# Attention and an MLP on one core: a third product with v in three passes, and what makes room for it

## The reference

```python
q_rot, k_rot = (rotate(q), rotate(k))                 # q, k, v: 4 x 8 heads x 576 x 64, fp32
scores = scale * np.matmul(q_rot, k_rot.transpose(0, 1, 3, 2))
scores = scores - np.max(scores, axis=-1, keepdims=True)
attn = np.exp(scores)
attn = attn / (np.sum(attn, axis=-1, keepdims=True) + 1e-09)
x = np.matmul(attn, v)                                # to (2304 tokens, 512)
h = x @ w_in                                          # 512 x 1024
e = np.exp(h - np.max(h, axis=-1, keepdims=True))
solu = h * e / (np.sum(e, axis=-1, keepdims=True) + 1e-09)
ln = (solu - mu) / np.sqrt(var + 1e-06) * g_ln
out = ln @ w_out                                      # 1024 x 512
```

## Time and profile before

| what | us |
|---|---|
| median of 3 runs | 485.28 (484.88 to 485.31) |
| the profiled execution's own time | 485.69 |
| its span | 483.6 |
| PE busy in the span | 474.4 |
| DVE busy | 375.4 |
| ACT busy | 263.7 |
| POOL busy | 221.7 |

### The profile page before, as it was taken

One profiled execution on the slowest core, in us unless ns is written; L12 is line 12 of the kernel. 1 busy time (PEld: TensorE's weight loads), 2 busy tenths in 40 slices (PEclk: granted clock), 3 DMA queues, 4 the chain that ended last, 5 costly groups with the idle time before them and its releaser, 6 DMA issues.

```text
span 483.6 us, 7879 instructions
## 1 busy us (share of the span) xinstructions
PE 474.4 (98%) x2555; PEld 402.4 (83%) x2555; DVE 375.4 (78%) x592; ACT 263.7 (55%) x398; POOL 221.7 (46%) x283
## 2 busy tenths in 40 slices
PE   7899999999999999999999999999999999999997
PEld 6678888988898888889888878888888888888885
DVE  6867887888879788878886366999997899888731
ACT  4667787777787778877786343032224222322221
POOL 6778565757575756666571012343343121122110
PEclk9999999999999999999999999999999999999999
DMA  8403455545454555445434203233333223322232
GB/s 289 186 18 76 139 159 112 175 136 169 101 152 150 150 143 148 148 115 179 123 80 100 58 15 58 32 82 67 86 69 80 47 50 69 84 54 62 60 78 86
DMA packets 101008, 50.60 MB, mean 105 GB/s; under 512 B 90280, under 2 KB 90280, under 8 KB 99048
## 3 DMA queue, kind: packets, MB, share of 16 engines
q1 hardware_dynamic: 100152, 50.00, 38.6%
q10 hardware_dynamic: 816, 0.10, 0.1%
HBM read 33.33 MB, written 4.79 MB: 79 GB/s over the span
## 4 chain that ended last, share of the span: by engine, by line
PE 94%; DVE 2%; DMA 1%; ACT 1%; issue 0%; SPq 0%; DVEq 0%; ACTq 0%
PE ps L1145 20%; PE ps L1159 20%; PE ps L1131 19%; PE ps L1082 18%; PE ps L1053 8%; PE ps L1111 5%; PE ps L1097 4%; DMA X<-x_in 1%; DVE nm L822 1%; DVE QK L797 1%; ACT p_main L633 0%; DVE X L763 0%; ACT QK L580 0%; DVE w_lo L846 0%; DVE X L768 0%
## 5 line engine op out<-in xcount | busy, mean ns | idle before, releaser
L822 DVE TENSOR_REDUCE nm<-ps 128x1 fp32r<-128x576 f32 x144 | 108.0, 755 | 34.0 <-PE ps L1053 31.8
L1131 PE MATMUL ps<-p_main,V 128*128 128x288 f32 x400 | 113.6, 406 | 0.0
L1145 PE MATMUL ps<-w_hi,KB 128*128 128x512 f32 x288 | 91.4, 390 | 0.0
L1159 PE MATMUL ps<-w_hi,QK 128*128 128x512 f32 x288 | 91.0, 389 | 0.0
L1082 PE MATMUL ps<-QK 128*128 128x288 f32 x320 | 89.0, 359 | 0.8 <-ACT p_main L633 0.5
L633 ACT ACTIVATE p_main<-ps 128x576 f32<-128x576 f32 x100 | 65.1, 651 | 36.4 <-PE ps L1082 34.7
L409 POOL TENSOR_TENSOR X<-X,rope 128x1152 f32<-128x1152 f32 x26 | 68.6, 2662 | 32.9 <-DVE KB L807 32.7
L1131 PEld LDWEIGHTS ps<-p_main,V 128*128 128x128 f32 x400 | 70.2, 189 | 10.7 <-ACT p_main L633 0.2
L1082 PEld LDWEIGHTS ps<-QK 128*128 128x128 f32 x320 | 55.3, 189 | 18.4 <-issue 5.7
L1082 PE MATMUL ps<-KB 128*128 128x288 f32 x320 | 67.8, 293 | 0.0
L654 ACT ACTIVATE X<-ps,neg_max 128x1024 f32<-128x1024 f32 x18 | 20.1, 1118 | 84.5 <-DVE neg_max L867 84.5
(11 more groups left out here) (114 smaller groups left out, 726.9 us busy)
## 6 DMA issues: line engine op xcount, KB each, us to landing
X<-x_in SPq DMA_DIRECT2D x13, 1152.0 KB, 5.2
V<-oe SPq DMA_DIRECT2D x213, 32.0 KB, 1.9
V<-v_in SPq DMA_DIRECT2D x32, 160.0 KB, 2.7
out<-X SPq DMA_DIRECT2D x18, 256.0 KB, 2.3
w_raw<-w_in SPq DMA_DIRECT2D x16, 256.0 KB, 3.0
xT<-x_in SPq DMA_DIRECT2D x2, 1152.0 KB, 10.8
xT<-oe SPq DMA_DIRECT2D x16, 144.0 KB, 2.4
inv<-inv_rows SPq DMA_DIRECT2D x16, 144.0 KB, 3.0
```

Source lines behind the costliest of these rows:

```text
L822: nc.vector.tensor_reduce(nm[g][:, at:at + 1], src[:, :, 0:HALF], AX_XY, ALU.max, negate=True)\
L1131: ins = nc.tensor.matmul(o_ps[a][:, half, 0:HALF], v, p[:, half * HALF:(half + 1) * HALF], start=(k == 0), stop=(k == 9))
L1145: ins = nc.tensor.matmul(h_ps[t % 3][:, half, :], left[a][:, c, :], right[:, col:col + 512], start=(c == 0 and k == 0), stop=(c == KC - 1 ...
L1159: ins = nc.tensor.matmul(y_ps[a], left[a][:, c * P:(c + 1) * P], right[:, col:col + 512], start=(i == 0), stop=(i == DOWNS - 1))
```

## The change

`HALVED` gets a third member, k=1, head A's second product, from pair 2 to pair 14. `p_hi` and `p_lo` stay one tile each; the halves of v get a tile for each member. For this:

- step 1's exponential goes to head B's bank, so in pairs from 2 on `take_o(n - 1, 1)` is issued ahead of it, not behind it;
- step 3's exponential waits for product 1, whose `p_hi` it overwrites;
- VectorE does `low_p(n, 1)` in step 1, and from pair 2 on no longer `low_queries(n + 1, 1)`, which GpSimd does at the head of pair n, ahead of the rotation;
- GpSimd halves v for k=1 and k=3 ahead of the division, for k=8 behind it;
- two more constants are set at the start.

```diff
-HALVED = (3, 8)
+HALVED = (1, 3, 8)
@@ halved
-            return k in HALVED and 1 <= n < PAIRS - 1
+            return k in HALVED and (2 if k == HALVED[0] else 1) <= n < PAIRS - 1
@@ GpSimd, halve_v(m, k)
+                i, a = HALVED.index(k), head(k)
+                first = 2 if i == 0 else 1
                 pool.wait_ge(v_loaded[m % 2], uses(m) * 32)
-                if m >= 2:
-                    pool.wait_ge(pv_done, PVS * (m - 1) + HALVED[a] + 1)
-                    pool.wait_ge(v_lo_done[a], m - 1)
+                if m > first:
+                    pool.wait_ge(pv_done, PVS * (m - 1) + k + 1)
+                    pool.wait_ge(v_lo_done[i], m - first)
@@ GpSimd, start
-            pool.wait_ge(v_const, 8)
+            pool.wait_ge(v_const, 10)
@@ GpSimd, pairs
             for n in range(1, PAIRS):
+                if n == 1:
+                    pool.wait_ge(low_q_done[1], 3)
+                elif n + 1 < PAIRS:
+                    pool.wait_ge(low_k_done[1], n + 2)
+                    pool.wait_ge(hi_done[1], high(n + 1, 1))
+                    pool.wait_ge(low_q_done[1], n + 1)
+                    low_queries(n + 1, 1)
+                    pool.wait_ge(low_q_done[1], n + 2)
                 if n + 2 < PAIRS:
-                    pool.wait_ge(low_q_done[1], n + 2)
...
-                if halved(n + 1, HALVED[0]):
-                    halve_v(n + 1, 0)
+                for k in HALVED[0:2]:
+                    if halved(n + 1, k):
+                        halve_v(n + 1, k)
                 if n >= 2:
                     divide(n - 2)
-                if halved(n + 1, HALVED[1]):
-                    halve_v(n + 1, 1)
+                if halved(n + 1, HALVED[2]):
+                    halve_v(n + 1, HALVED[2])
@@ ScalarE
+                    if s == HALVED[1] and n >= 2:
+                        act.wait_ge(pv_done, PVS * n + HALVED[0] + 1)
...
                 for s in range(STEPS):
+                    if s == 1 and n >= 2:
+                        take_o(n - 1, 1)
                     exp(n, s)
...
-                        if s == 1:
-                            take_o(n - 1, 1)
+                        if s == 1 and n == 1:
+                            take_o(0, 1)
@@ VectorE
-                    if s == 1:
-                        low_queries(n + 1, 1)
+                    if s == 1 and halved(n, HALVED[0]):
+                        low_p(n, HALVED[0])
+                    if n == 1 and s == 1:
+                        low_queries(2, 1)
```

More of the change, by code:

```diff
@@ L89, in attention_then_mlp @@
         p_lo = sb("p_lo", [P, S], F32R)
-        v_hi = [sb(f"v_hi_{h}", [P, P], F32R) for h in "ab"]
-        v_lo = [sb(f"v_lo_{h}", [P, P], F32R) for h in "ab"]
+        v_hi = [sb(f"v_hi{i}", [P, P], F32R) for i in range(len(HALVED))]
+        v_lo = [sb(f"v_lo{i}", [P, P], F32R) for i in range(len(HALVED))]
         oe = [sb(f"oe{c}", [P, 2, S]) for c in range(2)]
@@ L104, in attention_then_mlp @@
         p_lo_done = sem("p_lo_done")
-        v_hi_done = [sem(f"v_hi_{h}_done") for h in "ab"]
-        v_lo_done = [sem(f"v_lo_{h}_done") for h in "ab"]
+        v_hi_done = [sem(f"v_hi{i}_done") for i in range(len(HALVED))]
+        v_lo_done = [sem(f"v_lo{i}_done") for i in range(len(HALVED))]
         second_done = sem("second_done")
@@ L217, in halved, with halves, head @@
         def halved(n, k):
-            return k in HALVED and 1 <= n < PAIRS - 1
-        def halves(n, a):
-            return 2 * (n - 1) + a + 1
+            return k in HALVED and (2 if k == HALVED[0] else 1) <= n < PAIRS - 1
+        def halves(n, k):
+            i = HALVED.index(k)
+            return i if n == 1 else 3 * (n - 2) + i + 3
+        def head(k):
+            return k // 5
         def high(m, a):
@@ L439, in set_tails, with halve_v @@
                 pool.wait_ge(tails_set, 3 * m)
-            def halve_v(m, a):
+            def halve_v(m, k):
+                i, a = HALVED.index(k), head(k)
+                first = 2 if i == 0 else 1
                 pool.wait_ge(v_loaded[m % 2], uses(m) * 32)
-                if m >= 2:
-                    pool.wait_ge(pv_done, PVS * (m - 1) + HALVED[a] + 1)
-                    pool.wait_ge(v_lo_done[a], m - 1)
[L447 to L452, removed]
+                if m > first:
+                    pool.wait_ge(pv_done, PVS * (m - 1) + k + 1)
+                    pool.wait_ge(v_lo_done[i], m - first)
+                v = V[m % 2][:, a, (k - 5 if a else k + 1), own(a)]
+                nc.gpsimd.tensor_copy(v_hi[i][:, own(a)], v).then_inc(v_hi_done[i], 1)
+                pool.wait_ge(v_hi_done[i], m - first + 1)
+                nc.gpsimd.tensor_tensor(v_lo[i][:, own(a)], v, v_hi[i][:, own(a)].bitcast(F32), ALU.subtract)\
+                  .then_inc(v_lo_done[i], 1)
+                pool.wait_ge(v_lo_done[i], m - first + 1)
             def second_queries(m):
@@ L494, in _ @@
                 nc.gpsimd.memset(V[c][:, 1, :, 0:D], 1.0).then_inc(v_const, 1)
-            for a in range(2):
-                nc.gpsimd.memset(v_hi[a][:, other(a)].bitcast(F32), 1.0).then_inc(v_const, 1)
-                nc.gpsimd.memset(v_lo[a][:, other(a)].bitcast(F32), 0.0).then_inc(v_const, 1)
-            pool.wait_ge(v_const, 8)
+            for i, k in enumerate(HALVED):
+                nc.gpsimd.memset(v_hi[i][:, other(head(k))].bitcast(F32), 1.0).then_inc(v_const, 1)
+                nc.gpsimd.memset(v_lo[i][:, other(head(k))].bitcast(F32), 0.0).then_inc(v_const, 1)
+            pool.wait_ge(v_const, 10)
             nc.gpsimd.memset(expo[:, :], -0.5).then_inc(const_done, 1)
@@ L544, in _ @@
             pool.wait_ge(low_q_done[0], 3)
-            halve_v(1, 0)
-            halve_v(1, 1)
+            halve_v(1, HALVED[1])
+            halve_v(1, HALVED[2])
             for n in range(1, PAIRS):
+                if n == 1:
[6 more added lines that the diff above has]
+                    pool.wait_ge(low_q_done[1], n + 2)
                 if n + 2 < PAIRS:
-                    pool.wait_ge(low_q_done[1], n + 2)
                     if n == 1:
@@ L830, in row_max, with low_p @@
                     nc.vector.transpose(nm_row[g][:, :], nm[g][:, :].bitcast(F32)).then_inc(turned[g], 1)
-            def low_p(n, a):
-                dve.wait_ge(p_hi_done, halves(n, a))
+            def low_p(n, k):
+                a = head(k)
+                dve.wait_ge(p_hi_done, halves(n, k))
                 nc.vector.tensor_tensor(p_lo[:, :].rearrange("p (b c) -> p b c", b=2), o_ps[1 - a][:, :, 0:HALF],
@@ L949, in _ @@
                         low_keys(n + 1, 1)
-                    if s == 1:
-                        low_queries(n + 1, 1)
+                    if s == 1 and halved(n, HALVED[0]):
+                        low_p(n, HALVED[0])
+                    if n == 1 and s == 1:
+                        low_queries(2, 1)
                     if s == 4 and n >= 2:
                         w_low(n - 1)
[L954 to L957, removed]
+                    if s == 3 and halved(n, HALVED[1]):
+                        low_p(n, HALVED[1])
+                    if s == 7 and halved(n, HALVED[2]):
+                        low_p(n, HALVED[2])
                     if s == 5 and n + 2 < PAIRS:
@@ L1101, in weigh_tails, with weigh_halves @@
                             ins.then_inc(pv_done, 1)
[L1103 to L1109, removed]
+            def weigh_halves(n, k):
+                i, a = HALVED.index(k), head(k)
+                pe.wait_ge(v_lo_done[i], n - 1 if i == 0 else n)
+                pe.wait_ge(p_hi_done, halves(n, k))
+                for part, (v, p) in enumerate(((v_hi[i], p_hi), (v_lo[i], p_hi), (v_hi[i], p_lo))):
+                    if part == 2:
+                        pe.wait_ge(p_lo_done, halves(n, k))
                     for half in range(2):
@@ L1117, in weigh @@
                     if half == 1:
-                        weigh_halves(n, k // 5)
+                        weigh_halves(n, k)
                     return
@@ L1124, in weigh @@
                         pe.wait_ge(v_loaded[c], uses(n) * 32)
-                        pe.wait_ge(v_const, 8)
+                        pe.wait_ge(v_const, 10)
                         pe.wait_ge(max_taken, STEPS)
```

## The result

The changed kernel takes 488.81 us (median of 6 runs, 488.31 to 489.28), the kernel before 485.29 in the same comparison (484.88 to 485.66). The ratio is 1.0067, 95% interval 1.0056 to 1.0078: 3.5 us slower, where 3.3 were forecast.

What follows compares the result with a forecast made beforehand. TensorE, busy 98% of the span, bounds the kernel. 12 x 0.28 - 0.04 = +3.3 us on 485.28 gives 488.6 us, range 484.4 to 490.6.

Steps and rivals of the forecast that it cites:

- line 2: At each pair's end, GpSimd's third halving delays the division, which holds VectorE's low queries: 0.28 us more a pair, 12 times.
- the stall: TensorE's rows(1) wait for VectorE's delayed maximum of step 0: 0.46 us a pair.
- swap: Product k=1 as six matmuls (0.79 us) instead of four fp32 ones (0.97): at most 0.18 us gained in 13 pairs.
- Rival B: GpSimd and VectorE share the port, not held: at half pace L807 ends 0.31 us later, 484.8 us; chance 0.28.
- line 1: Step 1's chain of copy-out, exponential, p_hi, p_lo, third pass: p_lo late, leaving 0.04 us of 0.18 a pair.
- Rival D: GpSimd's halving for k=8 slips in ahead of L807: 0.32 us more a pair, 492.4 us; chance 0.03.
- C: ScalarE doesn't overlap its two copies, 13 x 0.09 = 1.2 us, and GpSimd's third halving is harmless: 486.5 us; chance 0.07.
- a dependent instruction starts 0.03 behind: On ScalarE in step 1, the exponential starts 0.03 us after the copy-out ends, at 155.68 after 155.65.
- the cover of the rotation: GpSimd's rotation, delayed by head B's low queries, ends about 163.2, one us before VectorE's addition at 164.2: no cost.

Runs made afterwards that it cites:

- before_spare_halving: The kernel before with one more, unused halving on GpSimd ahead of the division in pairs 3 to 14: 490.76 us, ratio 1.0112.
- division_first: The changed kernel with the division in front of both halvings on GpSimd: 485.57 us, ratio 1.0006 to the kernel before.
- division_last: The changed kernel with the division behind all three halvings and GpSimd going on only when it is done: 491.82 us, ratio 1.0143.
- one_more_halving: The changed kernel with an unused halving ahead of the other two, so the division comes later still: 489.73 us, ratio 1.009.
- scalar_reordered: division_first with ScalarE's head B second-query copy moved to step 2 and key copy to step 5: 486.58 us, ratio 1.0026.
- copy_out_first: The kernel before with only head B's copy-out moved ahead of step 1's exponential: 485.61 us, ratio 1.0006.
- before_early_addition: The kernel before with the addition in step 4, w_low in step 5, split high copy, head B's low queries on GpSimd: 484.6 us, ratio 0.9983.
- late_pass: division_first with the third pass of k=1 issued behind scores(3): 486.1 us, ratio 1.0016.

## Why the prediction was right, point by point

**The one forecast mechanism is the one that acted.** Each step of line 2 has its row. The division starts 0.47 ahead of L826 (predicted 0.44), keeps its 1.43, and L826 ends 0.60 after it (0.61). L826 is 1.56 long in the place where 1.60 were predicted. rows(1) come 0.47 late (0.46), in pairs 3 to 14 and not in pair 2. The pair is 16.83 to 16.86, but for one (16.84). Two runs take the steps apart: the stall alone, with no swap, costs 5.5 us (before_spare_halving), and the change without the stall costs nothing (division_first). They close the sum: the stall of 0.46, less the 0.18 of three passes that run in full behind it, is 0.28 a pair, and the changed kernel is 0.27 a pair over division_first, where the swap is worth nothing.

**Rival B, the shared port, is excluded.** It had L807 end before 171.3 and the change gain 0.5 us or more. In every case where one of the two ran into the other, the later one ended a fixed time after the first: VectorE's 0.60 or 0.61 behind GpSimd in the changed kernel, in division_last (held 1.86) and in one_more_halving. Half pace gives no such fixed rest. The three operations lay beside what was left of the division for 0.96, 1.25 and 0.59 us; at half pace they would have ended 0.27, 0.13 and 0.46 behind it, where 0.60 and 0.61 were measured. And the division never got longer when it came first. The Trainium skill, GPSIMD Engine Reference, Key points, has the contention for VectorE instructions with two SBUF inputs, and the traces agree on which are hit: low queries, low keys and w_low are, p_lo with one PSUM input took its 0.76 beside the rotation. (In B's own sum, half of the 0.99 from 169.88 to 170.87 is 0.50 and not 0.43, and a stall of 0.18 means an end at 171.20, not 171.3; neither changes what it forecasts, since line 1 still covers it.) Rival D (a cast slipping in) did not happen either; C's line 1 was worse than forecast, but line 2 was not harmless.

**What was off: line 1's spacing.** The step "a dependent instruction starts 0.03 behind", taken from an exponential and its p_hi, doesn't hold for a copy-out and the exponential behind it. These stand 0.71 to 0.77 apart in every kernel that has this order (0.68 taken). That makes p_lo late enough that the three passes take 0.95, and the swap is worth 0 a pair and not 0.04. It changed nothing in the forecast, since the stall of line 2 covers line 1 in the 12 pairs, but it is why division_first came out at 485.57 and not at 484.8. The longer spacing isn't due to the work ahead (scalar_reordered) nor to the exponential's writing to PSUM (copy_out_first). It goes with the wait: step 6's exponential stands behind head A's copy-out and doesn't wait for it. In before_early_addition it starts 0.57 behind in 11 pairs, as soon as its scores are there (164.56 in TensorE's chain) and while the copy-out still has 0.06 to go:

```profile
164.03 0.63 ACT L655 ACTIVATE oe<-ps 128x576 f32<-128x576 f32 x1
164.60 0.65 ACT L647 ACTIVATE p_main<-ps 128x576 f32<-128x576 f32 x1
```

Why an exponential that waits starts 0.09 to 0.12 behind the copy-out's end, where p_hi starts 0.03 behind the exponential's, stays open. In the code three waits stand ahead of this exponential and one ahead of p_hi; no run varied that.

**What was off: the cover of the rotation.** The prediction gave the rotation "one us of cover", counted to the addition at 163.93. In VectorE's order `w_low` comes before it (162.59 in the kernel before), and by the prediction's own rule it is held too, having two inputs in SBUF. In the changed kernel it lasts 0.95 to 0.98 instead of 0.75 in 10 of the 11 pairs that rotate from pair 3 on, and in pair 8 the cover that is left is 0.10. The term was rightly put at nothing there, but by little; in pair 6 it was not.

**The sum.** Medians differ by 3.52, the sum said 3.3. From the tails of pair 1 to those of pair 14 the two traces differ by 3.58 (215.69 and 219.27). That is not the same amount in each pair: from tails to tails 11 of the 12 are 16.83 to 16.85 long, 0.28 more than before as forecast, and the one with pair 6's late rotation is 17.12. 12 x 0.28, 0.28 more for that one and 0.06 less up to pair 2, which has line 1 alone, make the 3.58. The spans of the two profiled executions differ by only 3.1, since the changed kernel reached the tails of pair 1 0.66 earlier in its own.

**What I missed in the experiments.** Four of them lost to a wait that I had not followed far enough: past the rotation to w_low, which is itself a two-input operation (division_last, one_more_halving), from p_lo to the exponential of step 2, for which scores(3) then stood idle for 0.20 (late_pass), and from the moved key copy to the high copy and the maximum, for which rows(8) stood idle for 0.21 (scalar_reordered).

## What to carry to other kernels

Work added to an engine with time to spare isn't free if it shifts when that engine's long instructions start: 0.7 us on GpSimd, busy 46%, cost TensorE 0.46 a pair. List GpSimd's operations and VectorE's with two SBUF inputs in order of time, and keep them from meeting just ahead of an instruction for which the bound engine waits; the first try is to move the long one ahead of the short ones, which cost a swap of two statements here and returned 3.2 us. An exchange that saves 0.18 on TensorE pays only if the last result it needs, here p_lo, is there in time: look for that before writing the faster product. And cover is counted to the first operation that can be held, here `w_low`, not to the one that waits by name.

## What the runs showed of the hardware that was not expected

- One GpSimd operation can hold a VectorE operation for more than its own length: 1.86 us instead of 0.75 for the low keys beside a division. w_low beside the rotation took 0.95 to 1.40 instead of 0.75.
- It goes the other way too: a division of 1.43 took 1.81 when VectorE had started 0.25 before it.
- A copy-out and an exponential that waits for it stand 0.71 to 0.77 apart at 0.63 to 0.65 us each; an exponential that doesn't wait for the copy-out has started 0.57 behind it; an exponential and the p_hi that waits for it 0.67.
- A later division, by an unused halving, made VectorE's low queries short again (0.78) and the kernel still slow: the same 0.7 us of work cost 5.5 us in one kernel and 0.9 in the other.
